# A dummy indirect transfer before a scatter, and small VectorE work moved to ScalarE, in an attention + routed experts + MLP kernel

## The reference

```python
mask = q_bucket[:, :, :, None] == k_bucket[:, :, None, :]      # 8 heads of 64, hashed to 64 buckets
scores = np.where(mask, scale * q @ k.T, -1e9)
x = softmax(scores) @ v                                         # attention; rows of 8 x 64 = 512

logits = x @ w_gate                                             # 8 experts, top 1, capacity 192 tokens
expert_idx = np.argmax(logits, axis=1)
h = np.maximum(np.einsum('ecd,edf->ecf', disp, w1), 0.0)        # disp: each expert's tokens in order
y = np.einsum('ecf,efd->ecd', h, w2)                            # F = 1024
out[i] = gate_w[i] * y[expert_idx[i], pos[i]]

h = out @ w_in                                                  # 512 -> 2048 -> 512
g = h * np.tanh(softplus(h))
return g @ w_out
```

## Time and profile before

| | |
|---|---|
| median of 3 runs | 396.37 us (396.25, 396.37, 398.9) |
| the profiled execution's own time | 396.37 us |
| its span | 394.6 us |
| PE busy | 383.8 us (97%) |
| DVE busy | 281.3 us (71%) |
| ACT busy | 232.5 us (59%) |
| POOL busy | 116.1 us (29%) |
| granted TensorE clock over the span | 0.997 |
| the chain that ended last | PE 58%, DMA 3%, POOL 1%, issue 1% |

### The profile page before, as it was taken

How to read it: one execution, slowest core, us unless ns; L and a number is a source line. 1 busy time by engine, 2 the same in 40 slices (tenths; PEclk the granted TensorE clock), 3 DMA queues, 4 the chain that set the end, 5 groups by cost and what they waited for, 6 DMA issues and landing times.

```text
span 394.6 us, 6808 instructions
## 1 busy us (share of the span) xinstructions
PE 383.8 (97%) x2387; PEld 346.5 (88%) x2388; DVE 281.3 (71%) x446; ACT 232.5 (59%) x448; POOL 116.1 (29%) x122
## 2 busy tenths in 40 slices
PE   8999999999999999899999999999999999999995
PEld 3688999999999797889998999899899988999984
DVE  4888898899998626440447744569899998877861
ACT  5969869969887415530444654457666666544631
POOL 1853643742820160039999300000000000000015
PEclk9999999999999999999999999999999999999998
DMA  8684944974913347996797889090000000000004
GB/s 284 226 202 104 247 107 124 295 157 100 420 43 130 140 162 258 391 359 225 272 359 294 287 336 360 0 304 18 1 2 0 2 0 2 1 0 2 0 5 159
DMA packets 16092, 62.89 MB, mean 159 GB/s; under 512 B 2992, under 2 KB 3888, under 8 KB 11456
## 3 DMA queue, kind: packets, MB, share of 16 engines
q1 hardware_dynamic: 14560, 58.61, 44.3%
q0 software_dynamic: 992, 3.19, 2.1%
q10 hardware_dynamic: 512, 0.73, 0.6%
HBM read 49.89 MB, written 3.19 MB: 135 GB/s over the span
## 4 chain that ended last, share of the span: by engine, by line
PE 58%; DMA 3%; POOL 1%; issue 1%; SPq 0%; POOLq 0%; ACT 0%; DVE 0%; ACTq 0%
PE ps L1084 17%; PE ps L1109 16%; PE ps L957 13%; PE ps L1004 8%; DMA ring<-in_w 2%; PE ps L1025 2%; DMA rows<-xg,sloti 1%; PE ps L985 1%; POOL rows L664 0%; POOLq L102 0%; SPq L520 0%; POOL out L685 0%; DVE outs L1722 0%; ACT yh L1298 0%; ACT ysb L1292 0%
## 5 line engine op out<-in xcount | busy, mean ns | idle before, releaser
L957 PE MATMUL ps<-xs,ring 128*128 x512 | 60.6, 276 | 1.3 <-DMA ring<-in_w 1.3
L957 PEld LDWEIGHTS ps<-xs,ring 128*128 128x128 f32 x512 | 59.5, 191 | 2.0 <-issue 1.6
L1533 DVE TENSOR_TENSOR ptl<-ps,pth 128x384 fp32r<-128x384 f32 x96 | 49.0, 552 | 4.3 <-ACT pth L1237 3.7
L1237 ACT ACTIVATE pth<-ps 128x384 fp32r<-128x384 f32 x96 | 42.0, 490 | 15.9 <-PE ps L879 15.3
L1456 DVE TENSOR_REDUCE nmax<-ps 128x1 f32<-128x768 f32 x48 | 45.7, 955 | 4.8 <-PE ps L749 2.4
L681 POOL DMA_INDIRECT spare<-fold,toki x1 | 1.0, 1013 | 161.4 <-PE ps L1109 161.4
L749 PE MATMUL ps<-ops 128*128 128x384 f32 x192 | 44.3, 353 | 0.8 <-DMA ops<-qo 0.7
L1191 ACT ACTIVATE prob<-ps,nmax 128x768 f32<-128x768 f32 x48 | 43.5, 906 | 0.2 <-DVE nmax L1456 0.2
L1084 PE MATMUL ps<-yh,wih 128*128 128x384 f32 x128 | 43.0, 336 | 0.3 <-ACT yh L1298 0.3
L1084 PE MATMUL ps<-yh,wlow 128*128 128x384 f32 x128 | 42.9, 335 | 0.0
L1084 PE MATMUL ps<-yl,wih 128*128 128x384 f32 x128 | 42.0, 335 | 0.0
(11 more groups left out here) (191 smaller groups left out, 781.5 us busy)
## 6 DMA issues: line engine op xcount, KB each, us to landing
ring<-in_w SPq DMA_DIRECT2D x32, 1024.0 KB, 5.4
wraw<-in_w_in SPq DMA_DIRECT2D x2, 1280.0 KB, 8.4
wraw<-in_w_out SPq DMA_DIRECT2D x2, 1280.0 KB, 11.0
ops<-kh SPq DMA_DIRECT2D x12, 192.0 KB, 7.0
ops<-qh SPq DMA_DIRECT2D x6, 384.0 KB, 8.9
xg<-rows SPq DMA_DIRECT2D x3, 513.0 KB, 5.1
raw<-in_vt SPq DMA_DIRECT2D x4, 384.0 KB, 5.0
wraw<-in_w_in SPq DMA_DIRECT2D x6, 256.0 KB, 4.8
```

What stands on the lines that cost most here:

```text
L957: last = mm(ps[:, fc // 2, (fc % 2) * WIDE:(fc % 2) * WIDE + W], wa[:, 2 * fc // KF, kd, P * (fc % (KF // 2)):P * (fc % (KF // 2)) + P], x ...
L1237: av(pth[:, (n // HT) % 2, HT * b:HT * b + HT, n % HT, :], ps[:, tile_banks(n)[b], 0:HALF].rearrange("p (a c) -> p a c", c=P), ACT.Copy).t ...
L1533: V.tensor_tensor(ptl[:, m2, HT * b:HT * b + HT, u, :], ps[:, tile_banks(n)[b], 0:HALF].rearrange("p (a c) -> p a c", c=P), pth[:, m2, HT ...
```

## The change

Four edits.

- GpSimd: the zeroing of `xs`'s last columns goes, and in its place stands an indirect transfer to `spare`, with the token numbers just written to `xg` as its row numbers. Its semaphore `prime` is waited for only near the end of the program, before line 681.
- ScalarE: zeroes these columns (a copy of `iota` with scale 0) behind its last `ots` copy; scales the last head's rows itself, six tiles of 128x64 with `rinv` as the scale (`last_head`, three before and three behind the exponential); and then writes tile 0 of `xg` in one piece as the others (before: 448 columns, a wait, 64 columns). A new semaphore `lr` counts the six tiles, `lx` says that VectorE has read the logits of bank `XB`.
- VectorE: `scale_out(H - 1)` goes, and with it the wait behind it; the slots' conversion follows the first `hot` at once. It waits for `lr` before the bounds.
- TensorE: waits for `lr` where it waited for `fr` (one instruction, the last block of the first tile in line 933).

```diff
             nc.gpsimd.tensor_copy(xg[:, :, DM:DM + 1].bitcast(U32), c32("tok").unsqueeze(2)).then_inc(s["tokc"], 1)
-            nc.gpsimd.memset(xs[:, :, T:TPAD], 0.0).then_inc(s["zy"], 1)
             gp.wait_ge(s["tokc"], 1)
+            gp.indirect_dma_start(out=spare[:, :], out_offset=bass.IndirectOffsetOnAxis(
+                ap=xg[:, 0, DM:DM + 1].bitcast(U32), axis=0), in_=fold[:, 0:W72], in_offset=None).then_inc(s["prime"], 16)
             gp.wait_ge(s["si"], 1)
...
             gp.wait_ge(s["tokr"], 16)
+            gp.wait_ge(s["prime"], 16)
...
                 if t == 0 and kd == KD - 1:
-                    pe.wait_ge(s["fr"], 1 + H)
+                    pe.wait_ge(s["lr"], NT)
...
+            def last_head(tiles):
+
+                for t in tiles:
+                    av(xq[:, t, H - 1, :], ps[:, XB, W72 * t:W72 * t + D], ACT.Copy,
+                       scale=rinv[:, NT * (H - 1) + t:NT * (H - 1) + t + 1]).then_inc(s["lr"], 1)
+
+            act.wait_ge(s["cr"], 16)
+            act.wait_ge(s["vs"], NPAIR)
+            act.wait_ge(s["pa"], PA * (NPAIR - 1))
+            act.wait_ge(s["pd"], PD * (NPAIR - 1))
+            act.wait_ge(s["opsB"], DMASB * (NPAIR - 1))
+            av(xs[:, :, T:TPAD], c32("iota")[:, 0:WIDE].unsqueeze(1).to_broadcast([P, KD, WIDE]), ACT.Copy,
+               scale=0.0).then_inc(s["zy"], 1)
+            act.wait_ge(s["rc"], PAIRED + 2)
+            act.wait_ge(s["lx"], 1)
+            last_head(range(HT))
             act.wait_ge(s["g"], 1)
             av(small["ex"][:, :, :], small["df"][:, :, :], ACT.Exp).then_inc(s["gex"], 1)
+            last_head(range(HT, NT))
             act.wait_ge(s["gkr"], 1)
             act.wait_ge(s["fr"], H)
-            av(xg[:, 0, 0:DM - D], xq[:, 0, 0:H - 1, :].rearrange("p h d -> p (h d)"), ACT.Copy,
-               scale=col["gk"][:, 0:1])
-            act.wait_ge(s["fr"], 1 + H)
-            av(xg[:, 0, DM - D:DM], xq[:, 0, H - 1, :], ACT.Copy, scale=col["gk"][:, 0:1]).then_inc(s["xga"], 1)
-            for t in range(2, NT, 2):
+            act.wait_ge(s["lr"], NT)
+            for t in range(0, NT, 2):
...
                 if t == 0:
-                    scale_out(H - 1)
                     V.tensor_copy(sloti[:, :], co["slot"][:, :]).then_inc(s["si"], 1)
-                    dve.wait_ge(s["fr"], 1 + H)
+            dve.wait_ge(s["lr"], NT)
             dve.wait_ge(s["gpos"], 1)
```

More of the change, by code:

```diff
@@ L259, in attention_moe_mish @@
                   "pjh", "pjl", "wg",
-                  "S", "max", "P", "T", "hi", "lo", "PV", "OT", "os", "om", "xw", "fw", "fr", "pa", "pd", "vs", "rc", "tiny",
-                  "g", "gex", "ohm", "lth", "gt", "gm", "gpos", "gst", "gkr", "hotr", "xga", "xgd", "perm", "tokc", "tokr", "si", "sc", "back", "back2", "wide", "xw0", "xw1", "xt", "xa", "xd",
+                  "S", "max", "P", "T", "hi", "lo", "PV", "OT", "os", "om", "xw", "fw", "fr", "lx", "lr", "pa", "pd", "vs", "rc", "tiny",
+                  "g", "gex", "ohm", "lth", "gt", "gm", "gpos", "gst", "gkr", "hotr", "xga", "xgd", "perm", "tokc", "tokr", "prime", "si", "sc", "back", "back2", "wide", "xw0", "xw1", "xt", "xa", "xd",
                   "zy", "bnd", "Hw", "Ha", "Hd", "Yc", "Yw", "ya", "yd", "w2h", "w2l", "ye", "Ty",
@@ L1544, in _ @@
             dve.wait_ge(s["fw"], H)
-            link(V.tensor_tensor(sm["ex"][:, :, :],
-                                 ps[:, XB, 0:NT * W72].rearrange("p (t c) -> p t c", c=W72)[:, :, D:W72],
-                                 bc(rinv[:, NT * (H - 1):NT * H]), ALU.mult))
+            V.tensor_tensor(sm["ex"][:, :, :],
+                            ps[:, XB, 0:NT * W72].rearrange("p (t c) -> p t c", c=W72)[:, :, D:W72],
+                            bc(rinv[:, NT * (H - 1):NT * H]), ALU.mult).then_inc(s["lx"], 1)
+            dve.wait_ge(s["lx"], 1)
             link(V.tensor_tensor(sm["lg"][:, :, :], sm["lg"][:, :, :], sm["ex"][:, :, :], ALU.add))
```

## The result

The changed kernel takes 400.37 us (median of 6 runs, 400.02 to 401.72), the kernel before 396.69 in the same comparison (6 runs, 396.25 to 398.9): ratio 1.0086, interval [1.0064, 1.0109]. It is 0.9% slower, 3.7 us. The profiled execution took 400.52 with a span of 398.7, against 396.37 and 394.6. The forecast of 395.9 and its range up to 397.3 are both missed. The prediction took 1% for the least that a measurement can tell from no change; this interval tells 0.9%.

The account below looks back on a forecast made before the run. TensorE, busy 97%, was taken to be bound at two gaps by when expert 1's weights arrive behind the scatter. An earlier scatter gives both the same 0.47 us, once: 396.37 - 0.47 = 395.9 us, range 395.0 to 397.3.

Parts of the forecast that it names:

- the one on GpSimd and its sum: GpSimd's first scatter transfer starts at 136.81, ends at 138.95; the last starts 0.47 us earlier, giving 395.9 us.
- it ends between 135.2 and 136.35: Dummy on GpSimd, released at 133.89: starts 0.3 to 0.9 later and takes 0.96 to 1.52 us.
- I take 0, the transfers rule here: TensorE's line 933: the wait that goes is worth 0 to 0.1 us, counted as 0.
- Rival 3: Dummy still running at VectorE's first `hot`; real transfers queue behind it, the last 0.81 us later: 397.2 us; chance 0.18.
- the routing slips by up to 0.5: Alternative within rival 3: VectorE's `hot` waits for the dummy, delaying the routing by up to 0.5 us.
- VectorE's scaling goes, everything behind it 0.47 earlier: VectorE loses its 0.55 us scaling; the conversion moves from 136.54 to 136.07, all behind it by the same 0.47.
- ScalarE's part is hidden: ScalarE's zeroing (0 to 1.0 us) fits idle time; the exponential starts between 133.66 and 133.90, nothing lost.
- The late start, 0.60, is a first-time cost that the dummy takes: GpSimd's first scatter transfer starts 0.60 us late because it is the program's first; the dummy absorbs this.
- The long one, 0.56, is VectorE's doing: First scatter transfer takes 1.52 instead of 0.96 us because of VectorE's simultaneous SBUF-to-SBUF multiplies; the dummy won't shorten it.
- the single 0.12 of the trace before: First scatter transfer ended 0.12 us behind VectorE's multiplies (139.42 against 139.30), taken as evidence that they hold it.
- The last transfer 0.47 earlier: The scatter's last indirect transfer on GpSimd starts at 144.32 instead of 144.79.
- Both gaps of TensorE pay the same 0.47: Waits before expert 1 (160.18) and in its second layer (170.90) both end 0.47 us earlier, counted once.

Follow-up runs that it names:

- b_dummyonly: Kernel before with the dummy transfer alone added, zeroing of `xs` staying on GpSimd: 396.44 us, ratio 1.0013.
- h_before: Kernel before, repeated word for word on chip 1: 396.29 us, ratio 1.001.
- h_nodummy: Changed kernel without its dummy transfer, on chip 1: 397.62 us, ratio 1.0033 to the kernel before.
- j_late: Changed kernel with the dummy issued only once the counts of `gst` and `gpos` have been seen, on chip 8: 394.73 us, ratio 0.9959.
- f_early: Changed kernel with the dummy issued some 4 us before the routing matmuls, `toki` as indices: ratio 0.9959 on chip 10 (395.98 us), 1.0029 on chip 1 (397.45 us).
- m_small: Changed kernel with a dummy of 16 rows instead of 128, on chip 8: 394.62 us, ratio 0.9946.
- d_align: Changed kernel with scattered rows and `xg` padded from 513 to 544 floats, on chip 3: 399.17 us, ratio 1.0072.
- after: The changed kernel itself, as first measured and profiled against the kernel before: 400.37 us, ratio 1.0086.
- c_pewait: Changed kernel with TensorE also waiting for the last `perm` count before loading the bounds, on chip 3: 398.64 us, ratio 1.0065.
- a_nodummy: Changed kernel without its dummy transfer and the wait for it, on chip 3: 395.31 us, ratio 0.998 to the kernel before.
- n_late: j_late repeated word for word on chip 13: 400.34 us, ratio 1.008.
- l_behind: Changed kernel with the dummy moved from ahead of the scatter to behind it, on chip 8: 397.48 us, ratio 0.9994.

## Why the prediction was wrong

The step that failed is the one on GpSimd and its sum. It priced the dummy by what it does on POOL alone ("it ends between 135.2 and 136.35"), and took for TensorE that nothing changes ("I take 0, the transfers rule here"). What it left out is that counts of TensorE can come late beside indirect transfers. What the runs showed in place of that 0: `gst` counted 0.60 late, the last `perm` 4.10 late, a wait of TensorE of 3.67 us behind it, and 1.62 more for the lower clock. No rival had it. Rival 3 came nearest in place ("the routing slips by up to 0.5"; it slipped 0.58), but through VectorE, which only b_dummyonly shows (the `sume` of 0.84), and its dearest case was 0.81 us.

By its own steps:

- *VectorE's scaling goes, everything behind it 0.47 earlier.* Right, and cleanly so: counted from `ex`, the last transfer starts at 11.82 in h_before and at 11.36 in h_nodummy (chip 1, both with a first transfer of 1.15). That is the whole gain of the edits apart from the dummy.
- *ScalarE's part is hidden.* Right. The zeroing took 0.85 (bounds 0 and 1.0), and the exponential starts 1.08 behind `ex`, as before (133.66 - 132.58 and 133.89 - 132.81).
- *The late start, 0.60, is a first-time cost that the dummy takes.* Wrong. With a dummy 2.5 us earlier the first real transfer still starts 0.80 behind its tile of `xg` (written by ScalarE from 136.62 to 137.34, start 138.13), against 0.90 before. It is no first-time cost; these long starts stand where another engine ended the wait: j_late's dummy, too, starts 0.87 behind the count of `gpos` (134.65, 135.52), while the change's dummy stands 0.29 behind GpSimd's own cast. Worth 0.1, not 0.6.
- *The long one, 0.56, is VectorE's doing.* Wrong. In the change the first real transfer takes 0.96 from 138.13 to 139.09, while VectorE is within its `xg` multiplies from 138.39 on. By the prediction's reading, for which it had the single 0.12 of the trace before, it should have ended behind the last multiply, at 139.70 or later; the trace disagrees, and VectorE's three multiplies weren't held either (1.31 us, 1.27 before). The kernel before itself refutes it on chip 1: h_before's first transfer takes 1.15 and ends at 138.48, while VectorE multiplies until 138.73. What makes it 1.15 in one run and 1.52 in another stays open. Without a dummy the first takes 1.15 in four profiles and 1.48 to 1.52 in four; with one just ahead it takes 0.96 to 1.03, but then the second mostly takes 1.14 or 1.15; with one 6.9 us ahead (f_early) 1.16 again. The dummy so wins next to nothing against the first kind and 0.3 to 0.4 against the second.
- *The last transfer 0.47 earlier.* It came at 144.62, 0.17 earlier. Counted from `ex` it is 0.40, though the routing slipped 0.58: without the slip it would be about 11.23, and m_small, which has no slip, shows 11.27.
- *Both gaps of TensorE pay the same 0.47.* The reading of the gaps was sound: where no count is late, expert 1 still waits for its weights' DMA and starts earlier as the scatter does (27.60 to 25.85 in j_late, which includes a transfer time of 3.74 in place of 4.50). In the change TensorE comes to that place 5.24 us later (161.31 against 156.07), the weights have landed, and the wait is gone but for 0.41 on ScalarE's `xs`.

So the change costs 0.8 (routing) + 3.7 (the `xs` wait) + 1.6 (clock), less 2 that were waited for anyway. Shown: the late counts (seen in the records in three sets and the first comparison) and the waits that end with them, that `gst`'s goes with the dummy's place (of the twelve profiles with late counts six have a dummy over it and it is late, six don't and it isn't), that without the dummy 2.8 us of the loss on chip 1 are gone (400.42 and 397.62), and that the changed kernel is 0.8 to 1.0% slower on each chip on which it was run. On these three comparisons counts came late. On chips 10 and 8 none did, in eight profiles; the changed kernel itself was not run there, and its two nearest relatives without a further wait, f_early and m_small, were 0.4 and 0.5% faster than before. So I think, but have not shown, that it would be faster there.

Open: why some chips hold TensorE's counts (each chip was used in a single set, so an effect of the set can't be told from the chip's); whether recording has a part in it, since every time listed here comes with a recorded span and clock and half of the scatter's landing records are missing just where counts come late; and what sets a hold's length. So that the dummy makes the last hold longer is seen on chip 1 (4.11 with it, 2.82 without, nothing else changed, and no run of the one overlaps with the other's), but not how it does so. In all profiles with late counts but d_align the last late ones are raised 1.1 to 1.35 us after the last transfer of the scatter was issued and done on POOL (after: 146.74 against 145.58). But others come in the middle of the scatter, and c_pewait, with the dummy and the phase of the change, had 0.45: there TensorE stood still behind the group.

No version beats both kernels everywhere: j_late is 0.4% faster than before on chip 8 and 0.8% slower on chip 13; m_small was the fastest (0.9946), but was not run where counts come late. Of those run on a chip with late counts, a_nodummy is the best (0.998), and even it was 1.0033 on another.

## What to carry to other kernels

Indirect transfers on GpSimd may not be paid on POOL alone (here TensorE's counts came up to 4.40 us late beside them, and its waits were up to 3.71): before a dummy is put beside TensorE's work, ask which TensorE counts fall due while it and its neighbours run, and whether the critical path hangs on them. Look at the clock behind a long wait of TensorE too: in eleven profiles here the granted clock fell to 0.50 behind waits of 2.33 to 3.71 us (in n_late behind two, 1.33 and 2.45), in h_nodummy behind 2.49 it did not, and behind single waits of 1.63 and less never; in `after` that cost 1.62 us. And a kernel whose tight waits lie beside such transfers is to be measured on more than one chip, with unchanged copies among the experiments, before any edit is given the credit.

## What the hardware showed that I had not expected

- A matmul group's count was raised up to 4.40 us after the group had ended (n_late), while the recorded counts of VectorE and ScalarE in the same stretch come on time (b_dummyonly: one of ScalarE's due at 141.84 is 0.01 late, TensorE's that were due at 141.21 and 142.10 are 0.33 and 1.65 late). Such waits show in the profile as "remote" or "another core or an unknown queue" in a program of one core, or as a group that seems to last too long. The count is a thing apart from the group's modelled end: outside this stretch it comes 0.01 to 0.02 us behind it.
- It goes by chip: late in all twelve profiles of chips 3, 1, 13 and the first comparison, in none of eight on chips 10 and 8, with the same kernel (f_early) on either side.
- A dummy over 16 rows takes 1.06 us on POOL, one over 128 rows 1.14 to 1.19 ahead of the scatter, 0.95 right behind it (l_behind) and 1.01 near the end of the program.
